# Attention scores of two heads in the two row halves of TensorE, with head-major scratch, in a kernel of top-32 attention and two feed-forward layers

## The reference, cut to what matters

```python
# attention: q, k, v are (4, 8, 576, 64), float32
scores = (1 / 8) * np.matmul(q, k.transpose(0, 1, 3, 2))
kth = np.partition(scores, -32, axis=-1)[..., -32:-31]
scores = np.where(scores >= kth, scores, -1e9)
attn = softmax(scores)                       # with 1e-9 added to the sum
x = heads_side_by_side(np.matmul(attn, v))   # (2304, 512)
# layer 1: w_in (512, 2048), w_out (2048, 512)
h = x @ w_in
g = np.where(h >= 1, h, np.where(h <= -1, 0.0, (h + 1) ** 2 / 4))
x = g @ w_out
# layer 2, with weights of its own
out = np.maximum(x @ w_in2, 0) ** 2 @ w_out2
```

## Time and profile before

| | |
|---|---|
| median of three runs | 1234.5 us |
| the profiled execution's own time | 1234.88 us |
| its span | 1233.1 us |
| mean granted TensorE clock | 0.983 |
| busy: TensorE matmul, weight load | 1178.1, 1092.9 us |
| busy: VectorE, ScalarE, GpSimd | 839.2, 776.8, 740.9 us |
| DMA | 239.45 MB, 94914 packets |

### The profile page before, as it was taken

How to read it: one execution, slowest core, us unless ns; L and a number is a source line. 1 busy time by engine, 2 the same in 40 slices (tenths; PEclk the granted TensorE clock), 3 DMA queues, 4 the chain that set the end, 5 groups by cost and what they waited for, 6 DMA issues and landing times.

```text
span 1233.1 us, 23032 instructions
## 1 busy us (share of the span) xinstructions
PE 1178.1 (96%) x8184; PEld 1092.9 (89%) x8184; DVE 839.2 (68%) x1863; ACT 776.8 (63%) x1672; POOL 740.9 (60%) x589
## 2 busy tenths in 40 slices
PE   6777899999999999999999999999999999999998
PEld 4667888998889999999999999999999888998887
DVE  7999999999987799899899987878740111110000
ACT  7877666786765767767776665666654544653343
POOL 6868786888977767777676766665652222222222
PEclk9967999999999999999999999999999999999999
DMA  6767886777869932334458831456339500780000
GB/s 253 278 242 262 283 320 259 267 244 308 331 225 396 383 113 99 136 111 138 138 189 296 299 116 40 141 189 191 126 131 368 194 1 1 313 336 1 1 35 18
DMA packets 94914, 239.45 MB, mean 194 GB/s; under 512 B 7760, under 2 KB 46672, under 8 KB 82512
## 3 DMA queue, kind: packets, MB, share of 16 engines
q1 hardware_dynamic: 94640, 237.71, 53.4%
q10 hardware_dynamic: 160, 0.26, 0.1%
HBM read 166.12 MB, written 71.83 MB: 193 GB/s over the span
## 4 chain that ended last, share of the span: by engine, by line
PE 74%; POOL 9%; ACT 7%; issue 4%; DVE 3%; DMA 2%; SPq 1%; ACTq 0%; POOLq 0%
PE h_ps L691 22%; PE y_ps L725 11%; PE y_ps L719 10%; PE pv_ps L650 6%; PE score_ps L691 6%; PE tr_ps L623 4%; PE score_ps L588 3%; POOL s_sb L1232 3%; POOL prob L1237 3%; POOL kq_lo L1215 2%; PE y_ps L711 2%; PE y_ps L714 2%; PE tr_ps L714 2%; PE tr_ps L711 2%; DVE top L1054 1%
## 5 line engine op out<-in xcount | busy, mean ns | idle before, releaser
L691 PE MATMUL h_ps<-xt_ks,w_in 128*128 128x256 f32 (+1 forms) x2628 | 384.8, 296 | 2.2 <-ACT rg L931 1.4
L691 PEld LDWEIGHTS h_ps<-xt_ks,w_in 128*128 128x128 f32 x2628 | 341.8, 191 | 12.3 <-ACT rg L931 1.9
L1250 POOL TENSOR_TENSOR g_lo<-rg,g_hi 128x256 fp32r<-128x256 f32 x224 | 169.4, 756 | 281.6 <-ACT g_hi L949 165.8
L1054 DVE MAX8 top<-rest 128x8 f32<-128x576 f32 x432 | 304.5, 746 | 0.4
L1232 POOL TENSOR_SCALAR s_sb<-s_sb,top 128x576 f32<-128x576 f32 x126 | 222.1, 1763 | 33.8 <-DVE top L1054 33.8
L1056 DVE MATCH_REPLACE8 rest<-top,rest 128x576 f32<-128x576 f32 x288 | 211.4, 741 | 0.0
L1237 POOL TENSOR_TENSOR prob<-s_sb,prob 128x576 f32<-128x576 f32 x128 | 183.0, 1432 | 14.9 <-ACT s_sb L842 3.1
L719 PE MATMUL y_ps<-g_hi,w_out 128*128 128x256 f32 x896 | 180.9, 285 | 4.9 <-POOL g_lo L1250 4.5
L725 PE MATMUL y_ps<-w_out,g_hi 128*128 128x512 f32 x448 | 158.6, 395 | 0.8 <-ACT moves L910 0.7
L719 PEld LDWEIGHTS y_ps<-g_hi,w_out 128*128 128x128 f32 x896 | 147.6, 192 | 7.0 <-POOL g_lo L1250 5.7
L650 PE MATMUL pv_ps<-v_sb,pt 128*128 128x65 f32 x1024 | 129.9, 283 | 0.0
(11 more groups left out here) (122 smaller groups left out, 1819.9 us busy)
## 6 DMA issues: line engine op xcount, KB each, us to landing
w_in<-w_scratch SPq DMA_DIRECT2D x32, 1024.0 KB, 7.1
w_out<-w_scratch SPq DMA_DIRECT2D x32, 1024.0 KB, 8.2
xt_ks<-kq_scratch SPq DMA_DIRECT2D x46, 576.0 KB, 6.4
qs_g<-kq_scratch SPq DMA_DIRECT2D x152, 128.0 KB, 4.2
w_scratch<-w_in SPq DMA_DIRECT2D x16, 1024.0 KB, 7.3
w_scratch<-w_out SPq DMA_DIRECT2D x16, 1024.0 KB, 7.0
v_sb<-in_vv_dram SPq DMA_DIRECT2D x48, 325.0 KB, 6.4
moves<-in_w_dram SPq DMA_DIRECT2D x27, 512.0 KB, 6.5
```

The costliest lines, as they stand in the source:

```text
L691: last = pe.matmul(h_bank(k), wi[:, f // 2, w, m, cols], x_part(k, x, m), start=(m == 0 and n == 0), stop=(m == KT - 1 and n == 2))
L1054: dve.max(best, src[:, :]).then_inc(rank_step, 1)
L1250: pool.tensor_tensor(lo_of(k), u_of(k), hi_of(k).bitcast(F32), ALU.subtract).then_inc(g_lo_done, 1)
```

## The change

The scratch keeps the heads one above the other: rows 0 to 63 are head 0, rows 64 to 127 head 1, both for keys and queries. `ks` and `qs` hold a high and a low plane over these 128 rows. A normal score group `t` is now half of the keys for *both* heads: six matmuls of 288 columns, each over 64 rows, three products (high x high, high x low, low x high) times two heads, a head in its own half of the rows and its own PSUM bank. The product low x low is no longer made. Packed scores take the same three products over 128 rows, six matmuls, and the keys' order is mended by three loads (`load_tail_ks`) in place of one. A query load is one DMA rather than two, `restack` two writes rather than three.

A copy of scores then writes half of each head's row. There are three pairs of score buffers rather than two, the copy waits for the masks of slot n-3, and the first search of slot n waits for both copies.

In addition the staging of blocks 4 to 15 moves from the end of SP's slot to behind its query load, one slot later (`STAGE_SLOT`); in slots 10, 12, 14 and 16 ScalarE makes the high part of the step before it splits kq and makes the second exponential; and in slots 11, 13, 15 and 17 VectorE does the middle `activate` one pair of searches later.

```diff
-STAGE_SLOT = [-1, -1, -1, -1] + [max(s, 0) for s in W_SLOT[0:12]] + [16, 16, 18] + [s - 1 for s in W_SLOT[19:]]
+STAGE_SLOT = [-1, -1, -1, -1] + [s + 1 for s in W_SLOT[0:12]] + [16, 16, 18] + [s - 1 for s in W_SLOT[19:]]
...
-    kq_dram = [scratch(f"kq_scratch{g}", [3, 2 * DIM, KQ]) for g in range(PREPS)]
+    kq_dram = [scratch(f"kq_scratch{g}", [2, P, KQ]) for g in range(PREPS)]
...
+        s_pairs = sb("s_pairs", [P, 3, 2 * SEQ])
+        s_sb = [s_pairs[:, i // 2, SEQ * (i % 2):SEQ * (i % 2 + 1)] for i in range(6)]
...
+        def in_halves(n):
+            return RAW_SLOTS <= n < NORMAL
...
-                sp.dma_start(kq_dram[g][2, :, SEQ:KQ], kq_hi[:, SEQ:KQ].bitcast(F32)).then_inc(restacked, 16)
...
             def load_ks(g, i):
                 sp.dma_start(ks[i][:, :, :].bitcast(F32),
-                             kq_dram[g][0:2, :, 0:SEQ].rearrange("x (d h) c -> (x d) h c", h=2)
+                             kq_dram[g][:, :, 0:SEQ].rearrange("x p c -> p x c")
...
+            def load_tail_ks(g, i):
+                sp.wait_ge(restacked, 16 * 2 * (PREP_ORDER.index(g) + 1))
+                for rows, to, cols in ((slice(0, DIM), slice(0, SEQ), slice(0, SEQ)),
+                                       (slice(DIM, P), slice(0, MAIN), slice(TAIL, SEQ)),
+                                       (slice(DIM, P), slice(MAIN, SEQ), slice(0, TAIL))):
+                    sp.dma_start(ks[i][rows, :, to].bitcast(F32),
+                                 kq_dram[g][:, rows, cols].rearrange("x p c -> p x c")
+                                 ).then_inc(ks_loaded[i], 16)
...
                 if RAW_SLOTS <= n + 2 < NORMAL:
                     load_slot_qs(n + 2)
+                for i in range(4, WBLOCKS):
+                    if STAGE_SLOT[i] == n:
+                        stage_block(i)
...
-                for i in range(2 * WBLOCKS):
+                for i in range(WBLOCKS, 2 * WBLOCKS):
                     if STAGE_SLOT[i] == n:
                         stage_block(i)
...
-                    for var in range(2):
-                        for half in range(2):
-                            last = pe.matmul(score_ps[:, 512 * half:512 * half + HALF], qq[:, t, var, :],
-                                             kk[:, t, HALF * half:HALF * (half + 1)],
-                                             start=(var == 0), stop=(var == 1))
+                products = ((0, 0), (0, 1), (1, 0))
+                    for i, (x, y) in enumerate(products):
+                        for h in range(2):
+                            rows = slice(DIM * h, DIM * (h + 1))
+                            last = pe.matmul(score_ps[:, 512 * h:512 * h + HALF], qq[rows, x, :],
+                                             kk[rows, y, HALF * t:HALF * (t + 1)],
+                                             start=(i == 0), stop=(i == 2))
...
             def copy_scores(n, t):
                 u = 2 * n + t
-                if u >= 4:
-                    act.wait_ge(masked, u - 3)
+                if n >= 3:
+                    act.wait_ge(masked, 2 * (n - 3) + 2)
...
                 copy_at(q)
+                if n in PREP_SLOT and n in SINGLE:
+                    hi_at(q)
                 if n in SINGLE or q < UP_POS[0]:
                     split_new(n)
                 if here:
                     exponentiate(n, 1)
-                hi_at(q)
+                if n not in PREP_SLOT or n not in SINGLE:
+                    hi_at(q)
...
-                    dve.wait_ge(s_copied, 2 * n + t + 1)
+                    dve.wait_ge(s_copied, 2 * n + (2 if in_halves(n) else t + 1))
...
-                    if op == (6 if n in PREP_SLOT else 4) and n < DEFERRED[0]:
+                    if op == (6 if n in PREP_SLOT else 5 if n in SINGLE and n - 1 in PREP_SLOT else 4) \
+                            and n < DEFERRED[0]:
                         activate_at(3 * n + 1)
```

More of the change, by code:

```diff
@@ L224, in build @@
         neg_max = [sb(f"neg_max{i}", [P, 2]) for i in range(2)]
-        prob = [sb(f"prob{i}", [P, 2 * (MAIN + P)]) for i in range(2)]
+        prob = [sb(f"prob{i}", [P, 2 * SEQ]) for i in range(2)]
         pt = sb("pt", [P, 2 * (MAIN + P)])
@@ L603, in score @@
-                        pe.matmul(score_ps[:, 512:512 + MAIN - HALF], qq[:, 1, var, :],
-                                  kk[:, 1, TAIL + HALF:SEQ],
-                                  start=False, stop=(var == 1), skip_group_check=True)
-                        last = pe.matmul(score_ps[:, 512 + MAIN - HALF:512 + HALF], qq[:, 1, var, :],
-                                         kk[:, 1, 0:TAIL],
-                                         start=False, stop=(var == 1), skip_group_check=True)
+                            last = pe.matmul(score_ps[:, 512 * half:512 * half + HALF], qq[:, x, :],
+                                             kk[:, y, HALF * half:HALF * (half + 1)],
+                                             start=(i == 0), stop=(i == 2))
@@ L795, in copy_scores @@
                     for half in range(2):
-                        last = act.activation(s_sb[1][:, HALF * half:HALF * (half + 1)], y_ps[half][:, 0:HALF],
+                        last = act.activation(s_of(1)[:, HALF * half:HALF * (half + 1)], y_ps[half][:, 0:HALF],
                                               ACT.Copy)
@@ L1297, in lay_out @@
         for hh in range(2):
[L1298 removed]
+            rows = tail_rows = slice(DIM * hh, DIM * (hh + 1))
             kh, qh = kt[:, 2 * p + hh], qt[:, 2 * p + hh]
@@ L1318, in lay_out @@
             vv[:, p, tail_rows, at + DIM] = 1.0
-    for hh in range(2):
-        kq0[:, DIM * hh:DIM * (hh + 1)] = kq[0, 0:RAW_SLOTS // 2, hh::2, 0:RAW]
+    kq0[:] = kq[0, 0:RAW_SLOTS // 2, :, 0:RAW]
     blocks = []
```

92 lines of the change are left out of this document (48 added, 44 removed).

## The result

The changed kernel takes 1242.97 us, the median of five runs (1241.49 to 1243.51), beside 1234.85 us for the kernel before in the same comparison: a ratio of 1.006, with a 95% interval of 1.0049 to 1.0071. It is slower, by more than the 0.2% that a measurement can tell. The forecast was 1238, slower. The profiled execution, at 1243.51 us the slowest of the five, has a span of 1241.7 us, 8.6 more than before; by the terms it was to be 3.5 more.

A forecast was written before the change was run, and what follows sets the result against it. VectorE bounds slots 4 to 17, TensorE slots 18 to 63 and the packed ones; +12.3 - 5.7 - 1.0 - 1.6 + 0.7 - 1.2 = +3.5 on 1234.88 gives 1238.4 us. Own range 1235 to 1248, full range 1217 to 1250.

The forecast's parts named there:

- rivals 1 and 2: Scores of slots 18 to 63: mode change cheap, faster, chance 0.38; or row halves do not overlap, 1260, chance 0.05.
- I take 0.33: Normal score group: changing between 64 and 128 rows, in and out together, costs TensorE 0.33 us.
- rival 1: Transition around L588, slots 18 to 63: mode change cheap at full clock, 1229 or, if free, 1217.5; chance 0.38.
- 0.21 more: Normal score half, slots 18 to 63: 0.53 - 0.12 + 0.33, so 0.21 us longer than now.
- +12.3: Slots 18 to 63: 92 halves x 0.21 = 19.3 us, less about 7 of idle filled, leaves +12.3 us.
- A later TensorE fills about 7 of it: Slots 18 to 63: of TensorE's 8.5 us of idle, about 7 is filled by the added work.
- The three loads of keys in place of one are issued a slot and more ahead: Packed slots: key loads come early enough; if that cover is gone, the price is one issue of 1.2 us.
- -5.7: Packed scores: ten matmuls per half become six, sixteen halves x 0.36 us, all on TensorE: -5.7 us.
- -1.0: Third pair of score buffers: removes ScalarE's mask waits of 3.5 us, slots 18 to 71; -1.0 us (ends 0 and -3.5).
- +0.7: Both copies before a search: slot 4's first search waits, +0.4, and slower scores at half clock, +0.3 us.
- Staging -1.6: Slots 4 to 17: staging behind the query load removes VectorE's copy waits in slots 6 and 8; -1.6 us.
- The high part and the moved operation -1.2: Slots 11, 13, 15, 17: the later operation removes VectorE's 0.31 us curve waits, -1.2 us; the earlier high part 0.

The follow-up runs named there:

- b_narrow: Kernel before, but the four matmuls of a normal score half read only 64 of the 128 rows: 1261.93 us, ratio 1.0214.
- a_one_head: Changed kernel, but only the first head's three matmuls of each normal half are issued: 1241.2 us, ratio 1.0036 to the kernel before.
- a_full4: Changed kernel, but a normal score half is four matmuls over 128 rows in place of six over 64: 1228.65 us, ratio 0.9947 to the kernel before.
- a_tail_early: Changed kernel, but loads for a packed slot stand on SP's queue before the output store: 1238.2 us, ratio 1.0026 to the kernel before.
- a_two_pairs: Changed kernel with two pairs of score buffers in place of three, copies waiting for both masks of slot n-2: 1334.36 us, ratio 1.0805 to the kernel before.
- b_stage: Kernel before with only the staging of blocks 4 to 15 moved behind the query load: 1234.81 us, ratio 0.9998.
- hybrid: Kernel before plus moved staging, high part and operation, and packed scores of six matmuls with early loads; normal scores unchanged: 1226.89 us, ratio 0.9930.
- a_three_writes: Changed kernel with the third scratch write put back and waited for, though nobody reads it: 1243.22 us, ratio 1.0067 to the kernel before.
- a_by_head: Changed kernel, but a half's six matmuls are issued three of one head, then three of the other: 1240.57 us, ratio 1.0042 to the kernel before.

## Why the prediction came out as it did

**The mechanism was right, and rivals 1 and 2 are out.** The scores of slots 18 to 63 decide, through the change between 64 and 128 rows. The step "I take 0.33" measured 0.336 (b_narrow), at 2.4 GHz, between 0.19 (all of it halves with the clock) and 0.38 (none does), and above the 0.29 at which rival 1 decides. "0.21 more" for a half measured 0.217. By the Trainium skill (TensorEngine Tiling (Array Packing), Key Properties) such a change drains TensorE; the trace agrees, with the 0.336 us. That three matmul times and no more pass was right too (a_one_head: 1.267 against 1.279). The reason given, that a matmul's tail hardly scales with the clock, put the value near the upper end; the value bears that out, though no run tested the tail alone. The term +12.3 is 11.7 by a_full4. So the forecast had the sign and the cause; it was 5.1 us short in the span, and the paragraphs below say where.

**Idle filled.** "A later TensorE fills about 7 of it" was not so: idle of TensorE went from 8.5 to 5.3 us by the windows, so 3.2 were filled. But its busy time rose by 16.3 us, not by the 92 x 0.217 = 20 that the halves in the middle give; where the other 3.7 stayed was not followed. Slots 24, 29 and 35, among others, read TensorE busy all through in both kernels and are as long as they were, so a full busy figure doesn't say that more work lengthens a slot. VectorE fills 97% or more of 14 of the 46 slots, cut at the first searches, not of 12. The two errors nearly cancel, which is luck.

**The step that failed: the three key loads.** "The three loads of keys in place of one are issued a slot and more ahead": that is true of most packed slots, not of slot 69, whose loads stand behind an output store that waits. 16 halves give 16 x 0.37 = 5.9 us, as predicted: a group went from 1.16 us to 0.79, from the first score to the first transpose here:

```profile
807.26 0.95 PE L627 MATMUL score_ps<-xt_ks,qs_g 128*128 128x288 f32 x6
808.05 0.60 PE L644 MATMUL tr_ps<-ident,prob 128*128 128x128 f32 x4
```

Slot 69 took 4.0 of that back: -2.1 in place of -5.7. This alone is 3.6 of the 5.1 us by which the forecast was short. The text named the price if the cover is gone, "one issue of 1.2 us". The issues behind the store came 0.6 and 2.0 us later for the two halves; the rest of the price is loads that took longer to land and 1.5 us of TensorE at 1.2 GHz behind the wait, neither of which was in the text. In the four other kernels with this order of loads the same slot cost 0.7 to 2.5 us, so 4.0 is this execution's size and not the kernel's for certain. That the order is the cause, a_tail_early shows.

**Third pair of score buffers.** The wait that "-1.0" was to take away did go (3.5 us to none), but no gain shows: slots 18 to 63 are 1.4 us longer than before even with full-height scores (a_full4), almost all in slots 22 and 23, and those are longer in b_narrow too, which has no third pair. What the pair is worth in the changed kernel is another thing: copies that write both heads' rows need both masks, and without it 91 us are lost (a_two_pairs). The prediction did not price that condition. VectorE's waits for score copies in slots 18 to 63 rose from 2.4 us in 3 places to

```profile
DVE top L1082 <- ACT s_pairs L824: 8.4, 7, 1.9
```

**Both copies before a search.** +0.7 forecast, +1.1 measured in slots 0 to 3, of which 0.48 is the wait: b_narrow, without it, reaches slot 4 0.6 us later than the kernel before as well. VectorE waits at slot 4 as said, where the earlier trace rows has no wait:

```profile
47.72 1.42 DVE L1082 MAX8 top<-s_pairs 128x8 f32<-128x576 f32 x2 [0.48 <-ACT s_pairs L824]
```

**Slots 4 to 17.** -2.8 forecast, -3.5 measured, and -5.1 in the four kernels without a late stretch at half clock (149.0 us). Staging -1.6 forecast, -2.0 by b_stage. The high part and the moved operation -1.2 forecast, -3.1 from b_stage (152.1) to hybrid (149.0), and for another reason than the one given: the waits for the curve grew, and VectorE's instruction went from 711 to 443 ns, since GpSimd's low part no longer runs beside it. That the high part "lets GpSimd start its low part before the kq split" stood in the prediction, at 0. The waits that now stand there:

```profile
DVE rg L1145 <- ACT rg L967: 3.4, 3, 1.7
DVE top L1082 <- ACT s_pairs L824: 0.5, 1, 0.5
```

The first is 1.7 us in a_tail_early: half of it is the stretch at half clock. The second row shows that the copies of slots 6 and 8 are no longer late, as forecast.

**Writes and query loads** at 0 stand for the whole time; the third write is 0.9 us in slots 0 to 3 (a_three_writes). The DMA traffic fell from 239.45 to 224.25 MB and from 94914 to 74498 packets, and no stage shows a gain from it. The sum by stage, 11.7 + 1.4 (slots 18 to 63) - 2.1 + 1.1 - 3.5, is the 8.6 us; the 1.5 us of half clock in slot 69 and about as much in slots 4 to 17 are in it.

## What to carry to other kernels

Count how often a matmul stream changes between tiles and the full array before packing products into row halves: in this kernel a change in and out costs 0.34 us, so a group must save more than that, and here six half-height matmuls in place of four full ones save 0.12. Changing height is worth it for long runs of one kind, or where three products are enough over the full array, as in the packed slots. And a load's distance from its use is read in its own queue, slot by slot: one store that waits ahead of it, in one slot of eight, took more than half of a gain, and loads behind such a store can meet a slow landing and a fallen clock besides.

When one buffer comes to hold the work of two, ask what frees it: each wait on it becomes the later of two.

Before a difference of 1 or 2 us in a stage is put down to an edit, compare the granted clock of the same windows, and a second trace with the same code in that stage if there is one. Here one stretch of 3.4 us at 1.2 GHz was worth as much as the edits under test.

## What the runs showed of the hardware that was not expected

- The cost of the change of height is almost the same at either clock level: 0.38 us in the earlier trace rows at 1.2 GHz, 0.336 at 2.4 GHz. The score group that follows L650 and precedes L691 gives both kernels at 1.2 GHz with the same matmuls: 1.99 us before (from 111.6), 2.37 in b_narrow (from 115.2), 0.385 more. Array cycles alone would halve it.
- TensorE begins matmuls of one row half beside those of the other whatever the order of issue: with three and three issued by half, the starts still stand in pairs 10 to 24 ns apart (a_by_head). It rests on the recorded starts.
- A VectorE operation with two SBUF operands is held by some GpSimd operations and not by others. By the Trainium skill (SBUF — State Buffer, "SBUF: two separate sides") such an operation and a GpSimd operation that reads SBUF take one port pair as an exclusive lock, and the second waits for the whole of the first. The trace agrees for GpSimd's tensor_tensor: in the kernel before all 23 of L1117's operations of 128x256 that begin while one runs (L1215, L1237, L1250) end 0.28 to 0.30 us after it, whatever is left of it, and take up to 1.77 us, where 37 with GpSimd idle take 0.40 to 0.43. It does not agree for tensor_scalar (L1232), which reads SBUF too: the 51 that begin beside it take 0.40 to 0.88 us, 0.41 in the median, and do not wait for its end. In slot 12, VectorE and then GpSimd:

```profile
135.79 0.40 DVE L1117 SCALAR_TENSOR_TENSOR rg<-rg 128x256 f32<-128x256 f32 x1
134.44 1.72 POOL L1232 TENSOR_SCALAR s_sb<-s_sb,top 128x576 f32<-128x576 f32 x1
```

- The granted clock fell to 0.50 behind a wait of TensorE of 2.23 us in the kernel after (864.9 to 868.3) and stayed at 1.00 behind one of 2.19 us in a_three_writes; the fall cost 1.5 us.
